# Products with the values in a fused attention and two-layer kernel: the seven terms of one sum written side by side

## The reference

```
q_d, k_d, v_d = mean over groups of 4 positions        # 144 pooled positions
out_up = repeat(softmax(q_d k_d' / 8) v_d, 4)           # pooled attention, dense
mask   = |i - j| < 4                                    # a band of 7 positions
out_local = softmax(where(mask, q k' / 8, -1e9)) v      # banded attention
x = (out_up + out_local) as 2304 rows x 512
x = rmsnorm(x) * g;  x = (silu(x w_gate) * (x w_val)) w_out      # 512 -> 1536 -> 512
h = x w_in;  out = (s * relu(h)^2 + b) w2_out                    # 512 -> 2048 -> 512
```

## Time and profile before

| | us |
|---|---|
| median of 3 runs | 1060.56 (1059.51 to 1061.64) |
| the profiled execution, its own time | 1061.16 |
| its span in the trace | 1059.4 |
| PE busy | 970.9 (92%) |
| DVE busy | 604.6 (57%) |
| ACT busy | 332.4 (31%) |
| POOL busy | 383.3 (36%) |

### The profile page before, as it was taken

One profiled execution on the slowest core, in us unless ns is written; L12 is line 12 of the kernel. 1 busy time (PEld: TensorE's weight loads), 2 busy tenths in 40 slices (PEclk: granted clock), 3 DMA queues, 4 the chain that ended last, 5 costly groups with the idle time before them and its releaser, 6 DMA issues.

```text
span 1059.4 us, 13211 instructions
## 1 busy us (share of the span) xinstructions
PE 970.9 (92%) x5080; PEld 786.6 (74%) x5080; DVE 604.6 (57%) x814; ACT 332.4 (31%) x722; POOL 383.3 (36%) x198
## 2 busy tenths in 40 slices
PE   3657677799899999999999999999999999999997
PEld 2545566798877767777776889787888888888896
DVE  6868976789568767866675222334343443343343
ACT  2334346322332243133323244423232232222222
POOL 3647753977286657747361045400000000000000
PEclk9999999899899999999999999999999999999999
DMA  9977433314041213201100334200100200010010
GB/s 241 257 186 195 142 119 100 108 53 128 18 132 55 65 53 100 87 25 39 57 25 1 119 131 129 80 1 28 52 1 0 80 1 1 20 41 1 1 41 21
DMA packets 54639, 77.65 MB, mean 73 GB/s; under 512 B 6224, under 2 KB 37936, under 8 KB 53680
## 3 DMA queue, kind: packets, MB, share of 16 engines
q1 hardware_dynamic: 52560, 72.09, 23.2%
q10 hardware_dynamic: 2016, 4.72, 1.2%
HBM read 66.17 MB, written 10.62 MB: 72 GB/s over the span
## 4 chain that ended last, share of the span: by engine, by line
PE 73%; DVE 9%; POOL 5%; issue 5%; DMA 4%; ACT 1%; SPq 1%; DVEq 0%; ACTq 0%; POOLq 0%
PE bank L609 23%; PE bank L717 6%; PE bank L718 6%; PE bank L719 6%; PE bank L735 6%; PE bank L736 6%; PE bank L737 6%; POOL prod L419 4%; PE bank L630 4%; PE bank L632 4%; PE bank L631 4%; DMA rawv<-in_v_dram 3%; DVE x L449 3%; DVE dv L1105 2%; DMA ks<-in_k_dram 1%
## 5 line engine op out<-in xcount | busy, mean ns | idle before, releaser
L419 POOL TENSOR_TENSOR prod<-qs,ks 128x896 f32<-128x896 f32 x80 | 174.2, 2200 | 108.0 <-DVE sc L439 71.8
L433 POOL TENSOR_TENSOR prod<-sc,vs 128x896 f32<-128x896 f32 x80 | 140.8, 1770 | 85.6 <-DVE x L449 61.1
L756 DVE SCALAR_TENSOR_TENSOR r<-bank,r 128x512 f32<-128x512 f32 (+1 forms) x80 | 51.1, 638 | 183.8 <-ACT r L744 183.8
L449 DVE TENSOR_REDUCE x<-prod 128x128 f32<-128x896 f32 x80 | 137.6, 1742 | 4.6 <-POOL prod L433 4.6
L719 PE MATMUL bank<-y_h,w2i_l 128*128 128x512 f32 (+1 forms) x320 | 117.7, 368 | 0.0
L630 PE MATMUL bank<-h_h,wo_h 128*128 128x256 f32 (+1 forms) x288 | 107.6, 373 | 1.0 <-ACT y_st L665 1.0
L651 DVE TENSOR_TENSOR bank<-bank,u 128x256 f32<-128x256 f32 (+1 forms) x72 | 40.5, 563 | 117.8 <-PE bank L609 109.2
L609 PE MATMUL bank<-x_h,wv_h 128*128 128x256 f32 (+1 forms) x288 | 104.3, 377 | 1.4 <-DVE h_l L657 1.4
L609 PE MATMUL bank<-x_h,wg_h 128*128 128x256 f32 (+1 forms) x288 | 93.3, 348 | 11.3 <-ACT u L639 11.3
L744 ACT ACTIVATE r<-bank 128x512 f32<-128x512 f32 (+1 forms) x80 | 44.4, 555 | 183.7 <-PE bank L719 183.1
L632 PE MATMUL bank<-h_h,wo_l 128*128 128x256 f32 (+1 forms) x288 | 97.9, 340 | 0.0
(11 more groups left out here) (118 smaller groups left out, 1971.1 us busy)
## 6 DMA issues: line engine op xcount, KB each, us to landing
raww<-in_moe_w_out_dram SPq DMA_DIRECT2D x14, 512.0 KB, 3.8
rawq<-in_q_dram SPq DMA_DIRECT2D x4, 1152.0 KB, 9.2
rawk<-in_k_dram SPq DMA_DIRECT2D x4, 1152.0 KB, 10.9
rawv<-in_v_dram SPq DMA_DIRECT2D x4, 1152.0 KB
ks<-in_k_dram SPq DMA_DIRECT2D x16, 280.0 KB
vs<-in_v_dram SPq DMA_DIRECT2D x16, 280.0 KB
raww<-in_moe_w_in_dram SPq DMA_DIRECT2D x8, 512.0 KB, 4.0
y_raw<-y_scr SPq DMA_DIRECT2D x4, 1024.0 KB, 4.9
```

Of the source, the lines that this page charges most:

```text
L419: pool.tensor_tensor(dst, qv, kv, ALU.mult).then_inc(prod_ready, 1)
L433: pool.tensor_tensor(dst, pv, vv, ALU.mult).then_inc(prod_ready, 1)
L449: dve.tensor_reduce(x[:, 2 * half:2 * half + 2, h * D:(h + 1) * D], over(prod[:, at_ % 2, :], [[BAND * D, 2], [1, D], [D, BAND]]), op=ALU. ...
```

## The change

In `pv_mult` POOL writes the product of position s, band place r and column d to place 448 s + d * 7 + r of the buffer, and no longer to 448 s + r * 64 + d. The inputs are read in the same order as before, so that successive results of one instruction lie 7 elements (28 bytes) apart, with 64 of them for each band place. In `pv_reduce` DVE reads the seven terms of one sum at a step of 1 and no longer at a step of 64; it reads the whole half in one go. The number of instructions, the buffers, the waits and the order on each engine stay as they are. `qk_mult` and `qk_reduce`, which use the same two buffers, are not touched.

```diff
@@ pv_mult
-            dst = over(prod[:, at_ % 2, :], [[BAND * D, 2], [D, BAND], [1, D]])
+            dst = over(prod[:, at_ % 2, :], [[BAND * D, 2], [1, BAND], [BAND, D]])
             pool.tensor_tensor(dst, pv, vv, ALU.mult).then_inc(prod_ready, 1)
@@ pv_reduce
             dve.tensor_reduce(x[:, 2 * half:2 * half + 2, h * D:(h + 1) * D],
-                              over(prod[:, at_ % 2, :], [[BAND * D, 2], [1, D], [D, BAND]]),
+                              over(prod[:, at_ % 2, :], [[BAND * D, 2], [BAND, D], [1, BAND]]),
                               op=ALU.add, axis=AX.X).then_inc(prod_used, 1)
```

## The result

| | us |
|---|---|
| after, median of 4 runs | 1049.54 (1047.47 to 1051.15) |
| before, median of 4 runs | 1061.10 (1059.51 to 1062.48) |
| ratio of after to before | 0.989, 95% interval 0.9867 to 0.9914 |
| the profiled execution of after, its own time | 1050.09, span 1048.3 |

The changed kernel is 1.1% faster, 11.6 us by the medians; the two profiled executions are 11.1 us apart. The granted clock of the whole profiled execution was 0.991 before and 0.995 after. All executions, of both kernels, count as fast ones.

What follows compares the result with a forecast made beforehand. DVE bounds the start; engines wait in turn in chunks 0 and 1; then PE is full. 6.0 + 4.2 + 1.0 = 11.2 us off 1061.16 gives 1050.0, median stated 1049.5; own range 1046 to 1053, over the cases 1046 to 1062.

Steps and rivals of the forecast that it cites:

- The sum, 1.08 us: DVE's L449, seven inputs side by side for each result: 1.08 us instead of 1742 ns, for all 80 sums.
- The product, 1.7 us and no more than 2.1: POOL's L433 with writes 28 bytes apart: median stays about 1.7 us; above 2.1 us the forecast is wrong.
- Rival 1: POOL's product costs 2.1 to 2.5 us, shrinking the gain in start and chunks: 1054 to 1057.4 us; chance 20%.
- rival 4: Slower: POOL's product costs 2.5 us or more, delaying chunks 0 and 1: 1071 at 3.0 us, 1079 at 3.38; chance 20%.
- Rival 3: DVE's sums of seven are not faster, with a restart for each result: 1060.5 us; chance 4%.
- rival 2: The start's gain disappears behind loads and PE; only chunks 0 and 1 and collisions gain: 1055.5 us; chance 8%.
- The start, 6.0 us: Tile 0, 99 to 175 us: shorter sums on busy DVE save 3.6 + 1.2 + 1.2 = 6.0 us.
- collisions: DVE and POOL two-input instructions holding each other up, at L331 and L499: at most 3.5 us gained, 1.0 taken.
- the forecast 0.7: In the start, new waiting of DVE for product 6, which moves forward less than its sum: about 0.7 us.
- Chunks 0 and 1, 4.2 us: 231 to 270 us, 8 steps: PE takes over the pace at 4.26 us a step, 34.1 instead of 38.3 us.
- Tiles 2 to 4, nothing: 48 of the 80 sums lie beside a full PE with steps of 8.2 us, so they gain nothing.

Runs made afterwards that it cites:

- third trace of the changed kernel: The changed kernel itself, unaltered, run again on a further chip as a standard: 1050.93 us, ratio 0.9908 to before; the traced execution took 1048.45 us.

## Why the prediction was right, point by point

**The sum, 1.08 us.** Right (1080 ns). Both the slope and the assumption that a result for every seven inputs is free held.

**The product, 1.7 us and no more than 2.1.** The median is 1.91 us, at the upper side of what the forecast allowed; in a row of ten products one takes 1.80 us (18.04 / 10). The reason was nearly the right one, but 1.89 ns an element was the whole instruction divided by 896, its fixed part with it. POOL's multiplications side by side take 0.93 us for 448 and 1.69 us for 896. That gives, as an estimate, 1.70 ns an element and a fixed part of 0.17 us, and a copy's write at a step of 7 then takes (1.04 - 0.17) / 448 = 1.94 ns. The write is 0.24 ns slower than the two reads, 0.2 us in 896, which is the size of what the median rose by. The writer-only run shows no cost in time.

**Rival 1, a product of 2.1 to 2.5 us, and rival 4, one of 2.5 us and more.** Neither came: the median is 1.91 us. The penalty of a write at a step is as large as rival 1 feared, 0.56 against 1.04 us in a copy of 448, but in the multiplication most of it is hidden. Rival 3 fell with the sum of 1.08 us, and rival 2 with the 4.6 us of the start.

**The start, 6.0 us.** Measured 4.6 from the minimum of batch 2 on. Up to the minimum at 129.42 it gained 0.8 us where 3.6 were forecast. The two sums behind it gained nothing and the next two 1.2 us, both as forecast. Behind sum 14 it gained 2.4 us, 0.6 from that sum and 1.8 from L331; the last sum's 0.6 us went to L491. The first of these stages is the step that failed. The seven sums did give 4.3 us of DVE's work. But collisions I looked for only between instructions with two inputs: L1114 has one, and waited 2.2 us for POOL's three products in a row, which seem to come in one piece because DVE now frees the buffers sooner. Product 6 was late by 0.93 us, near the forecast 0.7, and that is luck. Its sum was to move forward by 3.7 us and the product by 3.0. Counted from the minimum of batch 2, DVE was ready for it only 1.1 us earlier (24.96 against 26.11 us), and POOL began it 0.9 us later (24.05 against 23.20 us), behind the load of v, which came 1.2 us later and not 1.2 us earlier, and behind L921. In the third trace of the changed kernel there is no such wait. At the end of the start L331 fell from 3.37 to 1.61 us, while L491 rose to 1.84 (1.2 alone). The forecast of +1.0 for collisions was about 0.9 us of loss in its place (2.2 + 0.6 lost, 1.8 won in the start, 0.1 won at L499).

**Chunks 0 and 1, 4.2 us.** Measured 5.7. PE does set the pace, with L651 waiting for it at 246.10 and 258.86. I had counted 8 steps of 4.26 us from step 10, as if L651 stood in time with PE there. It was late: back from 246.10 by 5 steps of 4.25 us, PE had step 10's input ready at 224.85, and L651 ran at 226.28. DVE, now faster than PE, made up these 1.4 us as well: 34.1 - 1.4 = 32.7 against 32.58 measured.

**Tiles 2 to 4, nothing.** Right, shown by the run with these tiles alone.

**The time.** 1049.5 forecast, 1049.54 measured. The start and the collisions were forecast at 7.0 us together and measured 4.6, 2.4 too high; the chunks were 1.5 too low; and 0.8 us of the difference of the two executions lies outside the forecast terms (0.4 before the change acts, 0.4 behind step 6). So close an agreement is luck; the range of 1046 to 1053 is what the reasoning was good for.

## What to carry to other kernels

Let the side with slack pay for the step: a term of a sum that lies at a step of 4 or more elements of float32 costs DVE 0.67 us in 896, and a write at a step of 7 costs POOL 0.1 to 0.2 us in a multiplication of 896 with two inputs, though 0.41 to 0.48 us (in 448) in a copy. Count only the instructions that stand in a stage where their engine is waited for: 32 of 80 gave all of the gain that could be measured here. And where DVE and POOL work side by side, look at what each has next in its queue, since an edit that moves them by a microsecond can lose 2 us of its gain on an instruction of 16 elements. Two small changes of order were worth 3.6 us more here, together.

## What the runs showed of the hardware

- A float32 step of 2 elements (8 bytes) is free for reads of DVE (0.62 us for 448) and writes of POOL (0.58), a step of 4 costs the full price or nearly so (0.96 and 0.97), a step of 3 on DVE about half of it (0.78). The Trainium skill's page SBUF — State Buffer (§ Specifications (TRN2), cachelines) gives lines of 16 bytes with at least two hits for the full rate; both engines agree with it here.
- Some one-input instructions of DVE with SBUF on both sides wait for POOL as well: L1114 2.33 us beside three products, 0.16 alone. The Trainium skill's GPSIMD Engine Reference (§1, the row on SBUF interfaces) names DVE instructions in a 2-port mode or with two SBUF inputs; that L1114 runs in such a mode fits, but no run here shows its mode. The sums L449 and L439, which have one input too, kept their time beside POOL (min to max 1067 to 1094 and 1064 to 1089 ns).
- A POOL instruction can last until a DVE instruction is done that began after it. L921 began at 117.13 and ended 1.33 us after L331, which DVE started at 119.69; L919 took 4.59 us and L923 4.30 us in other runs and ended 1.33 and 1.34 us after an L331. But the place in DVE's queue does not decide it. With the reader alone L919 began 0.07 us after a sum L449, with one instruction between that sum and L331, and took 5.24 us; in the third trace of the changed kernel L921 began 0.06 us after such a sum in the same order, took 2.27 us and ended before L331 began. What decides it stays open.
- The granted clock from 0 to 180 us was about 0.57 in some profiled executions (0.59 and 0.56 in one of the changed kernel, with the first L651 at 170.71) and 1.00 in others (170.78). The times take no side. An execution whose mean clock over the whole span is about 0.92 has such a slow start in every trace that was kept; on four chips these executions of before had medians 0.8 us above, 2.1 and 1.0 us below and 0.1 us above the others (0.99).
- At the stall of step 7 of chunk 1, where PE waits, the clock fell in some traces. Before has 0.50 (the level of 1.2 GHz) from 275 to 280 us, at a cost of at most 0.4 us. One of the three traces of the changed kernel has 0.57 from 270 to 274 us, and its step 9 came 6.14 us after step 8, against 4.76 us in after at clock 1.00. That is 1.4 us, and may be part of why the changed kernel's runs lie further apart than those of before.
